# A fused attention, ELU block and gated experts kernel: gate logits in one burst turned by VectorE, second weights released by place, and accumulator adds moved ahead of splits

## What is computed

```python
scores = scale * q @ k.T                      # 4 batches, 8 heads, 576 positions, head size 64
scores = where((rel >= 0) & (rel < 64), scores, -1e9)
x = softmax(scores) @ v                       # laid out as 2304 tokens x 512
h = x @ w_in                                  # 512 -> 2048
x = where(h > 0, h, exp(min(h, 0)) - 1) @ w_out   # 2048 -> 512
logits = x @ w_gate                           # 8 experts
P = exp(logits - logits.max())
for _ in range(8):
    P /= P.sum(1) + 1e-9 ; P /= P.sum(0) + 1e-9 ; P *= N / E
out = sum(P[:, e] * (relu(x @ w1[e]) @ w2[e]) for e in range(8))   # 512 -> 1024 -> 512
```

## Time and profile before

| | |
|---|---|
| median of 3 runs | 1896.12 us (1891.44 to 1896.52) |
| the profiled execution | 1897.7 us |
| its span, first to last instruction | 1895.9 us |
| mean granted TensorE clock | 0.997 of full speed |
| PE busy | 1868.5 us, 99% of the span |
| DVE busy | 1498.8 us, 79% |
| ACT busy | 847.5 us, 45% |
| POOL busy | 647.8 us, 34% |

### The profile page before, as it was taken

One profiled execution on the slowest core, in us unless ns is written; L12 is line 12 of the kernel. 1 busy time (PEld: TensorE's weight loads), 2 busy tenths in 40 slices (PEclk: granted clock), 3 DMA queues, 4 the chain that ended last, 5 costly groups with the idle time before them and its releaser, 6 DMA issues.

```text
span 1895.9 us, 31366 instructions
## 1 busy us (share of the span) xinstructions
PE 1868.5 (99%) x11628; PEld 1831.6 (97%) x11628; DVE 1498.8 (79%) x1834; ACT 847.5 (45%) x1411; POOL 647.8 (34%) x513
## 2 busy tenths in 40 slices
PE   8989999999999999999999999999999999999998
PEld 6779999999999999999999999999999999999998
DVE  5777877878998888878878778788787787787877
ACT  6866655656664524333324233343333332432432
POOL 7733242333243343232332423332423324233220
PEclk9999999999999999999999999999999999999999
DMA  9983766663566766766666666667666666666654
GB/s 253 292 313 127 259 215 208 219 213 133 196 216 222 242 238 205 250 222 210 222 221 217 219 215 231 215 207 252 208 226 216 222 226 207 221 232 208 218 186 150
DMA packets 96653, 414.73 MB, mean 219 GB/s; under 512 B 9576, under 2 KB 10744, under 8 KB 96504
## 3 DMA queue, kind: packets, MB, share of 16 engines
q1 hardware_dynamic: 96504, 412.74, 64.1%
HBM read 374.88 MB, written 37.82 MB: 218 GB/s over the span
## 4 chain that ended last, share of the span: by engine, by line
PE 91%; DVE 4%; issue 2%; ACT 2%; POOL 1%; DMA 0%; ACTq 0%; DVEq 0%; POOLq 0%
PE ps L1350 29%; PE ps L1345 29%; PE ps L1352 29%; PE ps L1309 2%; PE ps L1325 1%; PE ps L1335 1%; DVE hb L1077 1%; DVE xs L966 0%; DVE ss L1009 0%; ACT ss L817 0%; DVE yacc L1104 0%; DMA x_store<-w2t 0%; PE ps L1302 0%; ACT pb L834 0%; ACT pb L829 0%
## 5 line engine op out<-in xcount | busy, mean ns | idle before, releaser
L817 ACT ACTIVATE ss<-hb 128x768 fp32r<-128x768 f32 x420 | 347.7, 843 | 596.0 <-DVE hb L1084 345.7
L1345 PE MATMUL ps<-xs,w1t 128*128 128x384 f32 x1680 | 563.8, 336 | 6.9 <-DVE hb L1077 2.0
L1345 PE MATMUL ps<-ss,w2t 128*128 128x384 f32 x1680 | 562.6, 335 | 5.7 <-DVE yacc L1104 5.2
L1350 PE MATMUL ps<-xs,w1t 128*128 128x384 f32 x1680 | 564.4, 336 | 0.0
L1350 PE MATMUL ps<-ss,w2t 128*128 128x384 f32 x1680 | 562.9, 335 | 0.0
L1352 PE MATMUL ps<-xs,w1t 128*128 128x384 f32 x1680 | 562.5, 335 | 0.0
L1352 PE MATMUL ps<-ss,w2t 128*128 128x384 f32 x1680 | 562.1, 335 | 0.0
L1104 DVE TENSOR_TENSOR yacc<-ps,yacc 128x768 f32<-128x768 f32 x396 | 377.7, 954 | 165.8 <-PE ps L1352 161.2
L1009 DVE TENSOR_TENSOR ss<-hb,ss 128x768 fp32r<-128x768 f32 x420 | 400.8, 958 | 22.2 <-ACT ss L817 12.3
L613 POOL TENSOR_TENSOR w1t<-wraw,w1t 128x512 fp32r<-128x512 f32 x140 | 187.6, 1354 | 484.8 <-DVE ss L1009 304.8
L613 POOL TENSOR_TENSOR w2t<-wraw,w2t 128x512 fp32r<-128x512 f32 x140 | 183.0, 1326 | 443.1 <-DVE hb L1032 230.8
(11 more groups left out here) (101 smaller groups left out, 1288.8 us busy)
## 6 DMA issues: line engine op xcount, KB each, us to landing
xs<-x_store SPq DMA_DIRECT2D x388, 768.0 KB, 4.3
wraw<-moe_w_dram SPq DMA_DIRECT2D x32, 1024.0 KB, 7.1
x_store<-xs SPq DMA_DIRECT2D x32, 768.0 KB, 3.8
pb<-p_store SPq DMA_DIRECT2D x24, 384.0 KB, 4.3
x_store<-w2t SPq DMA_DIRECT2D x10, 768.0 KB, 7.3
scratch<-q_dram SPq DMA_DIRECT2D x16, 288.0 KB, 5.5
scratch<-k_dram SPq DMA_DIRECT2D x16, 288.0 KB, 7.5
scratch<-v_dram SPq DMA_DIRECT2D x16, 288.0 KB, 8.3
```

What stands on the lines that cost most here:

```text
L817: nc.scalar.activation(ss[:, step, 0, :], hq(r, HOME[step]), ACT.Copy).then_inc(s_hi_done, 1)
L1345: nc.tensor.matmul(bank, w_parts[:, step, 0, cols], hi, start=step in FRESH and kt == 0, stop=False, skip_group_check=True)
L1350: nc.tensor.matmul(bank, w_parts[:, step, 0, cols], lo, start=False, stop=False, skip_group_check=True)
```

## The change

- **Gate.** The three hops of a window become one, in up step 1: 32 matmuls of 32 output columns over 96 tokens (`SQ` = 32 token squares), which leave in each quarter of the partitions the logits of other tokens, summed over all four input blocks by PSUM itself. DVE turns them by one transpose of 32 x 32 squares out of PSUM (`turn_logits`) and one copy into `gate`. `adder`, `move_parts`, `move_logits` and the matmuls with `adder` go. The maximum is taken in window 13, the shift is spread at its end, and the first two normalizing hops move from steps 4 and 6 of window 14 to steps 3 and 5.
- **Second weights by place.** `weight_hi(0, 1, step)` waits only for the staged pieces that lie where it writes; its step 0 moves ahead to attention step 50. The last input piece of chunks 0 and 1 is made one attention step earlier (9 instead of 10). The load of the raw first weights of group 1 moves from window 0 to window 1 behind the ring's load of that step.
- **Adds ahead of splits.** In every window DVE's `add_y(before, 1)` moves ahead of `lo(before, 4)`, and `add_y` of step 6 moves from the start of the next window to the end of its own; in windows 1 to 14 `add_c` of steps 4 and 5 go ahead of input pieces.
- **Round 1.** ACT's snapshots `snap_p1`, `snap_u2` and its first `copy_y` move ahead of the high parts that wait for DVE.
- Smaller moves of input sums in windows 1 and 2, and of `weight_sum_t4` around window 12.

The core of the diff:

```diff
-            for step, at in enumerate((0, 1, 4, 5, 6, 7, 10)):
+            for step, at in enumerate((0, 1, 4, 5, 6, 7, 9)):
...
-                    if step == 4 and c == 0 and g + 1 < GROUPS:
+                    if (w, step) == (1, 0) or step == 4 and c == 0 and 0 < g and g + 1 < GROUPS:
                         load_raw(g + 1, 0)
...
-                    for piece in STAGED[-STAGES:]:
+                    for piece in staged_in(step):
                         wait_x_stored(act, *piece)
...
+                if n == UNITS + 2:
+                    weight_hi(0, 1, 0)
...
+                if w == 1:
+                    snap_p1(r)
+                    copy_y(before, 0)
                 if down:
                     hi(before, 3)
...
+                if w == FIRST[CHUNKS - 1]:
+                    x_piece(1)
...
-                if w >= 2:
-                    add_y(w - 2, 6)
...
                 if up and w > 0:
                     add_c(r, 1, 1, H11)
+                    turn_logits(w)
+                if down:
+                    add_y(before, 1)
                 if down:
                     lo(before, 4)
...
-                x_piece(w, 3)
                 if up:
                     add_c(r, 4, 3, H22)
+                x_piece(w, 3)
...
+                if down:
+                    add_y(before, 6)
                 gate_work(w, 6)
...
+                        for kt in range(KT):
+                            for part in range(TT // SQ):
+                                square = slice(part * SQ, (part + 1) * SQ)
+                                nc.tensor.matmul(spare(w, step, j, HT, HT + HT * SQ // TT)[square, :]
+                                                 .rearrange("p (t n) -> p t n", n=SQ),
+                                                 wg[:, kt, :], tiles[:, kt, :, square], start=False,
+                                                 stop=kt == KT - 1, skip_group_check=True)
```

More of the change, by code:

```diff
@@ L86, in build_program @@
     for w, cc in [(1, 2)] + [(GATE_WINDOW + c, CHUNKS + c) for c in range(CHUNKS)]:
-        for at, step in ((3, 0), (4, 1), (6, 2)):
+        for at, step in ((3, 0), (4, 1), (5 if cc < CHUNKS else 6, 2)):
             XPREP[w][at].append((cc, step))
@@ L159, in build_program @@
         ones = sb("ones", [P, P])
-        wg = sb("wg", [P, KT, P // KT])
-        adder = sb("adder", [P, E])
+        wg = sb("wg", [P, KT, SQ])
         gate = sb("gate", [TT, E, TILES])
@@ L229, in x_home, with staged_in @@
             return xs[:, (STEPS * FIRST[cc] + k) % RING]
+        def staged_in(step):
+            first, last = 2 * WN * step, 2 * WN * (step + 1)
+            return [piece for n, piece in enumerate(STAGED[-STAGES:], len(STAGED) - STAGES)
+                    if n % STAGES * 2 * QN < last and (n % STAGES + 1) * 2 * QN > first]
         def rests(r, step):
@@ L350, in build_program, with logits_of @@
         stored = sem("stored")
-        GATE_TILES = {1: 4, 2: 0, 3: 2}
-        def logits_of(c, first, last):
-            t = c * CHUNK_TILES
-            return gate[:, :, t + first:t + last].rearrange("p e t -> p t e")
-        def summed(w, step, first, last):
-            return d_spare(w - 1, step, 0, E * first, E * last).rearrange("p (t e) -> p t e", e=E)
+        def logits_of(c):
+            return gate[:, :, c * CHUNK_TILES:(c + 1) * CHUNK_TILES].rearrange("p e t -> p t e")
         def unit(n, lag):
@@ L871, in weights @@
                             weight_hi(g, 0, STEPS - 1)
-                        else:
+                        elif w != GATE_WINDOW + 1:
                             weight_hi(g, 1, at - 1)
+                        elif at > 1:
+                            for step in (0, 1) if at == 2 else (at - 1,):
+                                weight_hi(g, 1, step)
                     if up and c == 1 and g > 0 and at == 0:
@@ L876, in weights @@
                     if up and w == 0 and at == 4:
-                        for i in range(3):
-                            weight_hi(g, 1, i)
+                        weight_hi(g, 1, 1)
+                        weight_hi(g, 1, 2)
                     if up and w == 1 and at < 4:
@@ L892, in _ @@
                 weights(0)
-                if up and w > 0:
+                if up and w > 1:
                     snap_p1(r)
@@ L897, in _ @@
                     hi(before, 5)
+                if w >= 2:
                     copy_y(before, 0)
                 x_piece(0)
+                if w == FIRST[CHUNKS - 1]:
+                    x_piece(1)
                 weights(1)
+                if w == MAX_WINDOW:
+                    act.wait_ge(shift_placed, 1)
+                    nc.scalar.activation(gate[:], gate[:], ACT.Exp, bias=gate_shift[0:TT, :]).then_inc(gate_exped, 1)
                 if down:
@@ L905, in _ @@
                     relu(r, 0)
+                if w == 1:
+                    snap_u2(r)
                 if up and w > 0:
                     hi(r, 0)
-                x_piece(1)
-                if w == MAX_WINDOW:
-                    act.wait_ge(shift_placed, 1)
-                    nc.scalar.activation(gate[:], gate[:], ACT.Exp, bias=gate_shift[0:TT, :]).then_inc(gate_exped, 1)
-                move_parts(w, 1)
+                if w != FIRST[CHUNKS - 1]:
+                    x_piece(1)
                 weights(2)
-                if up:
+                if up and w != 1:
                     snap_u2(r)
-                move_parts(w, 2)
                 if down:
@@ L955, in _ @@
             nc.vector.tensor_copy(maskb[:, 2:4, :], mask[:, 1:2, :].broadcast_to([P, 2, P])).then_inc(mask_placed, 1)
-            nc.vector.tensor_reduce(adder[:], ident[:].rearrange("p (k e) -> p e k", k=KT)[:, 0:E, :], AX.X, ALU.add) \
-                .then_inc(adder_made, 1)
             def x_lo(cc, k):
@@ L1224, in _ @@
                 gate_work(w, 1)
-                if up:
+                if up and w > 0:
                     lo(r, 0)
-                if down:
-                    add_y(before, 1)
                 gate_work(w, 2)
@@ L1438, in down_hop @@
             def down_hop(w, step):
-                if GATE_WINDOW <= w < MAX_WINDOW and step - 1 in GATE_TILES:
-                    pe.wait_ge(parts_placed, 3 * (w - GATE_WINDOW) + step - 1)
-                    for j in range(2):
-                        t = GATE_TILES[step - 1] + j
-                        nc.tensor.matmul(d_spare(w - 1, step, 0, E * t, E * (t + 1)), logit_parts[:, j, :], adder[:],
-                                         start=False, stop=True, skip_group_check=True)
-                if w == MAX_WINDOW - 1 and step == 5:
+                if w == MAX_WINDOW - 1 and step == 3:
                     pe.wait_ge(token_maxed, 1)
```

138 lines of the change are left out of this document (60 added, 78 removed).

## The result

| | before | after |
|---|---|---|
| median of 8 runs each | 1895.18 us (1891.44 to 1900.62) | 1887.99 us (1886.17 to 1890.72) |
| the profiled execution, its span | 1897.7, 1895.9 us | 1889.7, 1887.9 us |

The ratio is 0.9962, with a 95% interval of 0.9948 to 0.9977. The change is faster by 7.2 us, which is clear of noise though small (0.4%); the forecast was 15.8. The stretches of the changed kernel, cut as in the earlier trace rows at the first matmul of a window: length, busy us of PE, PEld, DVE, ACT and POOL, granted clock, DMA share, GB/s. The first row is all that comes ahead of window 0, the second window 0, then windows 1, 2, 3, 11, 12, 13, 14, 15 and 60; the last is a piece of attention, behind the wait at 84.08.

The account below looks back on a forecast made before the run. PE, busy in 99% of the span, bounds the kernel. Terms: 8.5 - 2.15 + 2.2 + 1.1 + 5.4 + 0 + 0.7 = 15.75, so median 1896.12 - 15.8 = 1880.3 us; range 1873 to 1889.

Parts of the forecast that it names:

- rival 1: Whole kernel, half a gain: staged store lands as late as before, split waits pull the clock down; 8 gained, 1888; chance 0.20.
- Attention, 2.15: Attention: last piece of chunk 0 delays the copy of unit 34, PE waits; with chunk 1's delay a loss of 2.15 us.
- What I kept as a bound: Attention: upper bound of the loss, 3.6 us, if the clock falls too behind the wait at unit 34.
- The 0.2 for chunk 1: Last piece of chunk 1 delays ACT's first snapshot and so up step 2 by about 0.2 us.
- Windows 0 and 1, 8.5: Windows 0 and 1: earlier store, ACT free 3.2 earlier, snapshot and `add_y` waits gone; gain 8.5 us, bounds 5 and 9.8.
- the bound of 9.8: Windows 0 and 1: upper bound of the gain, window 1's 8.29 and 1.5 at the turn into it.
- Window 2, 2.2: Window 2: up step 3's input piece still costs 1.4, the 0.5 wait ahead goes; gain 2.2 us, 1.0 if clock falls.
- rival 4: Window 1's waits only pass to window 2, DVE chain eats the gate's gain; 4 gained, 1892 us; chance 0.06.
- Window 3, 1.1: Window 3: its wait is for `add_y` of down step 1, which is now early; gain 1.1 us.
- Gate, 5.4: Windows 11 to 14: one burst replaces three hops; gains 2.05, 1.3, 0 and 2.1, sum 5.4 us, bounds 2 and 8.
- Every other window, 0: Some 50 windows with early `add_y` 1: DVE's idle 0.68 and 2.34 hide the delay; no change.
- Last window, 0.7: Last window: down step 1's 1.30 wait for `add_y` 6 shortens as that add runs first; gain 0.7 us.

## Why the prediction was wrong by half

The sign and most of the places that win were right, and the time of 1888 was in the range (rival 1 had the number, by other terms in part: its store did not land late); the forecast of 15.8 was twice what came. By its own steps:

- *Attention, 2.15.* Right, and too small. The wait at the values of unit 34 was 1.84 (at 84.08) for a forecast of 1.9, and the piece costs 1.9 in attention. What I kept as a bound happened: the clock fell to half behind it (0.65 from 84.08 to 89), 1.5 more; together 3.4. The 0.2 for chunk 1 came as 0.26, inside window 0. (That this difference can be read from two executions is luck: both reach the same place at 73.0 us, where others are up to 2.5 us later by their waits for loads and sums.)
- *Windows 0 and 1, 8.5.* Right in mechanism, won 9.9, just over the bound of 9.8. The last staged store landed 12.5 us after the start of window 0 for 17.4 before, and ACT went on with the second weights at 13.0, without idle time, where I had it at 14.3. Window 1 forecast about 30.5, measured 29.24: `act_f` 3 did not hold PE. Two of its causes are shown: the early add (4.9) and chunk 1's early piece (2.0). The release by place, the moved load and the snapshots were not undone one by one.
- *Window 2, 2.2.* **The step that failed most.** "The piece is ready at 13.9 where PE wants it at 12.5" took DVE to enter window 2 on time and each of its instructions to take 0.95. But window 1 now runs without PE waits and is 8.2 us shorter, so DVE has 4.1 us of its 10.2 of idle time left there, POOL's four sums for the next group and DVE's input work run beside each other, and DVE's instructions take up to twice as long. DVE enters window 2 with its activation late (0.92 at up step 1), and the piece comes at 15.9. Waits of 0.9, 2.1, 0.4 and 0.7 and a fall of the clock made 35.9 for 31.4. With POOL's work cut the piece comes at 13.7 and the window takes 31.96, near the forecast, part of it by the longer window 0 of that run; the order of the piece and the activation alone won nothing. That is rival 4's mechanism, waits of window 1 passed on, in part.
- *Window 3, 1.1.* The number came, the reason did not, so it came by luck: with the add back in place it stays at 29.12. What had brought its wait of 0.69 was not tried.
- *Gate, 5.4.* Window 11: 30.8, as forecast. The burst cost 1.67, worked out below, for 1.65. Windows 13 and 14 as forecast (waits of 1.27 and 1.23 for 1.4 to 1.6). Window 12 lost 0.9 for a gain of 1.3: "its `add_y` can start at 10.24" asked when PE was through, while DVE itself got there at 11.33, having been full since the window's start; and the burst waited 0.17 for `add_y` 6, so that up step 2 began at 10.50, for 10.00 in the runs without that wait. That, with waits of 1.9 and 0.36 at up steps 3 and 5, made 34.1 where the clock stayed up; the fall behind the 1.86 made 35.2 here. Here POOL was not the cause of the long wait, which stood with its work cut.
- *Every other window, 0.* True for the steady ones, and DVE's idle times ahead of the next two adds came out as forecast, none and 1.69 for the 0.68 and 2.34 of the earlier trace rows:

```profile
1007.20 0.95 DVE L1103 TENSOR_TENSOR yacc<-ps,yacc 128x768 f32<-128x768 f32 x1
...
1010.70 0.96 DVE L1103 TENSOR_TENSOR yacc<-ps,yacc 128x768 f32<-128x768 f32 x1 [1.69 <-PE ps L1357]
```

  Not true for window 15, which I had put at nothing without looking at its loads: stores that stand behind loads in SP's queue made it 1.1 longer.
- *Last window, 0.7.* Right.

So of the 7.8 us that were missing in the profiled execution, three falls of the clock make 3.5 (1.5, 0.9 and 1.1), window 2 without its fall 3.6 (34.96 for 31.4, which is 33.59 - 2.2), window 12 without its fall 1.1 (34.08 for 33.0), window 15 1.1 and windows 13 and 14 0.2, while windows 0 and 1 gave 1.4 back and attention without its fall 0.3: 7.8. The waits at unit 34 and in windows 13 and 14 came within 0.4 us of the forecast. What failed stands where DVE comes to its work late: in window 2 and in window 12.

The burst, by the timeline of PE in window 11, as in the earlier trace rows:

```profile
427.61 0.34 PE L1350 MATMUL ps<-xs,w1t 128*128 128x384 f32 x1
427.88 1.53 PE L1417 MATMUL ps<-yacc,wg 128*32 128x96 f32 x64
429.34 0.44 PE L1355 MATMUL ps<-xs,w1t 128*128 128x384 f32 x1
```

1.73 lie between two product matmuls that are 0.17 apart elsewhere, and the next comes 0.11 late: 1.67. Its 64 starts span 1.28 us: the four instructions that go to the four quarters start 6 to 7 ns apart, and from one such set to the next are 82 ns, for 109 ns in the hop of before with 128 columns. That is the 3/4 of 0.11 of the forecast. The 25 ns that the Trainium skill (TensorE: Matmul & The Clock Gate, section Wait — 56ns, not 53.3ns?) gives as the least from one start to the next is not kept here, with 6 to 7 ns inside a set and 20 on average; the 1.94 worked out from it was too high.

## What to carry to other kernels

When an order takes stalls out of one stage, cost the next stage anew: its helpers arrive together instead of one after the other, and two engines that share a way to memory slow each other just there. A queue that is busy for 97% of a window sets its own times; ask when the engine gets to an instruction, not when its input is ready. And a stage that gets shorter leaves less time for the loads and stores of the next, so follow those too.

## What was not expected of the hardware

A wait of PE of about 2 us is a draw. In the fourteen profiled executions of this study PE waited 27 times for 1.8 to 2.2 us; behind 18 of them the clock fell from 2.4 to 1.2 GHz for a while and behind 9 it did not, even at the same place and after the same wait: of the eight executions that waited 1.83 to 1.85 us at one place in attention, six show the fall. None of the 21 waits of 1.3 to 1.6 us was followed by a fall, and each of the three of 2.3 to 3.15 was (the wait of 5.6 us with which every execution begins is left out). A fall cost 0.9 to 1.5 us, the less where a wait for DVE further on took it up. So two executions of one kernel differ by one or two falls, and a span from one of them has to be read with its clock column.

DVE and POOL instructions that read two operands from SBUF at the same time took up to 2.05 us for 0.95 and 2.0 for 1.3. DVE instructions over 1.15 us held it 3.1 us longer than 0.955 each in window 1 and 3.0 in window 2 of the changed kernel, for 3.4 and 1.7 before.
